# Attention loads on two queues in a ring of six, stores per two tiles, weight splits moved to the experts

## The reference, cut to what matters

```python
def _attn_ref(r, k, v, w, u):            # (4, 8, 768, 48): batch, head, position, width
    for t in range(S):
        cur = einsum('bhd,bhe->bhde', u[None] * kt, vt)
        y[:, :, t] = einsum('bhd,bhde->bhe', rt, state + cur)
        state = w[None, :, :, None] * state + einsum('bhd,bhe->bhde', kt, vt)

def _moe_ref(x, w_skip, w_gate, w1, w2): # x (3072, 384), 8 experts, hidden 1024
    keep = x @ w_skip > 0; e = argmax(x @ w_gate)
    y = softmax(x @ w_gate)[e] * (maximum(x @ w1[e], 0) @ w2[e])
    return x + y where keep, x elsewhere

def _moe2_ref(x, w1, w2, w3, w_out):     # 384 -> 1024 -> 1024 -> 384
    return (((x @ w1) * (x @ w2)) @ w3) @ w_out
```

## Time and profile before

| quantity | value |
|---|---|
| median of three runs | 710.27 us |
| the profiled execution, whole | 708.51 us |
| its span, first to last instruction | 706.4 us |
| TensorE busy | 640.1 us (91%) |
| VectorE, ScalarE, GpSimd busy | 291.5, 224.4, 157.4 us |
| packets under 512 B, of all | 79875 of 106784 |
| mean granted TensorE clock | 0.954 |

### The profile page before, as it was taken

One profiled execution on the slowest core, in us unless ns is written; L12 is line 12 of the kernel. 1 busy time (PEld: TensorE's weight loads), 2 busy tenths in 40 slices (PEclk: granted clock), 3 DMA queues, 4 the chain that ended last, 5 costly groups with the idle time before them and its releaser, 6 DMA issues. The chain is left out here.

```text
span 706.4 us, 15335 instructions
## 1 busy us (share of the span) xinstructions
PE 640.1 (91%) x6244; PEld 571.7 (81%) x6244; DVE 291.5 (41%) x458; ACT 224.4 (32%) x400; POOL 157.4 (22%) x188
## 2 busy tenths in 40 slices
PE   7568687697899989899988899999999999999997
PEld 6457587686666989899987788888888889888886
DVE  5335465463291765566652212322322323213222
ACT  2224243342233544455541411321322213213221
POOL 7425464570254233222221400000000000000000
PEclk9877897897999999999999999999999999999999
DMA  6666667673460663566530300200200200100001
GB/s 123 126 146 124 154 127 158 157 170 117 132 248 17 199 207 124 206 209 211 201 123 19 134 1 1 89 1 1 90 1 1 89 1 1 45 1 16 31 0 45
DMA packets 106784, 67.87 MB, mean 96 GB/s; under 512 B 79875, under 2 KB 101541, under 8 KB 106737
## 3 DMA queue, kind: packets, MB, share of 16 engines
q1 hardware_dynamic: 104688, 62.62, 31.9%
q0 software_dynamic: 2048, 4.58, 1.9%
HBM read 56.31 MB, written 12.58 MB: 98 GB/s over the span
## 5 line engine op out<-in xcount | busy, mean ns | idle before, releaser
L1273 PE MATMUL gl_pab<-gl_xT_hi,wm_lo 128*128 128x512 f32 x288 | 112.9, 392 | 0.0
L1273 PE MATMUL gl_pab<-gl_xT_lo,wm_hi 128*128 128x512 f32 x288 | 112.8, 392 | 0.0
L1273 PE MATMUL gl_pab<-gl_xT_hi,wm_hi 128*128 128x512 f32 x288 | 112.1, 389 | 0.0
L1353 DVE TENSOR_TENSOR gl_g_sb<-gl_a_sb,gl_pab 128x512 f32<-128x512 f32 x48 | 33.0, 688 | 186.8 <-ACT gl_a_sb L1330 186.8
L1330 ACT ACTIVATE gl_a_sb<-gl_pab 128x512 f32<-128x512 f32 x48 | 28.7, 599 | 185.1 <-PE gl_pab L1273 185.1
L1288 PE MATMUL gl_po<-gl_wf_hi,gl_g_hi 128*128 128x384 f32 x192 | 65.6, 342 | 0.7 <-DVE gl_g_lo L1355 0.7
L1288 PE MATMUL gl_po<-gl_wf_hi,gl_g_lo 128*128 128x384 f32 x192 | 64.7, 337 | 0.0
L1288 PE MATMUL gl_po<-gl_wf_lo,gl_g_hi 128*128 128x384 f32 x192 | 64.5, 336 | 0.0
L1273 PEld LDWEIGHTS gl_pab<-gl_xT_hi,wm_lo 128*128 128x128 f32 x288 | 54.0, 188 | 11.4
L1273 PEld LDWEIGHTS gl_pab<-gl_xT_lo,wm_hi 128*128 128x128 f32 x288 | 54.0, 188 | 10.5
L1273 PEld LDWEIGHTS gl_pab<-gl_xT_hi,wm_hi 128*128 128x128 f32 x288 | 54.1, 188 | 10.3
(11 more groups left out here) (192 smaller groups left out, 1246.5 us busy)
## 6 DMA issues: line engine op xcount, KB each, us to landing
ew_w_in<-in_moe_w SPq DMA_DIRECT2D x16, 1536.0 KB, 6.8
k_in<-in_k SPq DMA_DIRECT2D x48, 96.0 KB, 2.9
r_in<-in_r SPq DMA_DIRECT2D x48, 96.0 KB, 3.0
v_in<-in_v SPq DMA_DIRECT2D x48, 96.0 KB, 2.9
xbuf<-x_nat SPq DMA_DIRECT2D x48, 96.0 KB, 2.3
gl_x_in<-xbuf SPq DMA_DIRECT2D x12, 384.0 KB, 4.0
out<-gl_o_sb SPq DMA_DIRECT2D x12, 384.0 KB, 2.6
w_in<-in_moe_w SPq DMA_DIRECT2D x8, 512.0 KB, 4.0
```

Source lines behind the costliest of these rows:

```text
L1273: m = pe.matmul(p_ab[f % 2][w][:, :], a[:, w * KD + k, cols], b[t.slot][:, k, :], start=(k == 0 and n == 0), stop=(k == KD - 1 and n == 2))
L1353: dve.tensor_tensor(g_sb[f % 2][:, :], a_sb[f % 2][:, :], p_ab[f % 2][1][:, :], ALU.mult).then_inc(s_g, 1)
```

## The change

1. The hardware loop in attention is gone: all 24 tiles are written out, with constant addresses and constant counts. TensorE's `ready()` (a semaphore increment that nothing waits for) goes too.
2. k, r and v have rings of six tiles (`NB = 6`). SyncE loads k and r of tile m+5. The v loads are issued by ScalarE: eight DMAs ahead of its first instruction, then two per step for tile m+5, behind `kT_out`.
3. `x_nat` holds two tiles per pair of batches; the store moves both, once per two tiles.
4. `v_in` loses its padding between heads and `k_rev` shares the memory of `A_m`.
5. The `wm` weights are loaded and split in the experts: with experts 0 to 5 one block of 128x1024 each, into the buffers `w3_in` of the fold. SyncE issues the load behind that of w2, ScalarE does `wm_hi` behind `x_hi`, GpSimd does `wm_lo` behind the gather.

```diff
-        def schedule(eng, parts, lead, lag, extra=None):
-            for n in range(-lead, NS):
-                step(n // NS, n % NS)
-            with eng.Fori(1, NCH - 1) as c:
-                for j in range(NS):
-                    step(c, j)
-            for n in range(NS * (NCH - 1), NT + lag):
-                step(n // NS, n % NS)
+        def schedule(parts, lead, lag, extra=None):
+            for m in range(-lead, NT + lag):
                 for f, shift in parts:
+                    if 0 <= m + shift < NT:
+                        f(Tile(m + shift))
...
             def load_rk(t):
-                wait(sp, s_Tr, t.num(1, 1 - NS))
+                wait(sp, s_Tr, t.n + 1 - NB)
...
-            def load_v(t):
-                wait(sp, s_Y, t.num(1, 1 - NS))
-                wait(sp, s_vb, t.num(1, 1 - NS))
...
-            def store(t):
-                wait(sp, s_x, t.num(1, 1))
+            def store(t):
+                if t.a == 0:
+                    return
+                sp.wait_ge(s_x, t.n + 1)
                 for jj in range(2):
-                    sp.dma_start(xbuf[bass.ds(t.chunk(P, C * t.a + (2 * t.pr + jj) * S), C), :], x_nat[t.pr][half(jj), :]).then_inc(s_store[t.pr], 16)
+                    sp.dma_start(xbuf[b * S + P * t.c:b * S + P * (t.c + 1), :].rearrange("(a s) w -> s a w", a=2), x_nat[t.pr][half(jj), :, :]).then_inc(s_store[t.pr], 16)
-            schedule(sp, ((load_rk, 4), (load_v, 3), (store, -2)), 4, 2, extra)
+            schedule(((load_rk, 5), (store, -2)), 5, 2, extra)
...
         def _(act):
+            def load_v(t):
+                wait(act, s_Y, t.n + 1 - NB)
+                wait(act, s_vb, t.n + 1 - NB)
+                for jj in range(2):
+                    act.dma_start(t.v(half(jj), 0, W).rearrange("p (h d) -> p h d", d=D), rows_of(v, t, jj)).then_inc(s_vin[t.buf], 16)
+            for n in range(4):
+                load_v(Tile(n))
...
-            schedule(act, ((kT_out, 1), (new_state, -1), (xT_out, -1), (y_out, 0)), 1, 2, extra)
+            schedule(((kT_out, 1), (load_v, 5), (new_state, -1), (xT_out, -1), (y_out, 0)), 1, 2, extra)
...
             def x_out(t):
-                wait(dve, s_store[t.pr], t.chunk(64, 32 * t.a))
+                wait(dve, s_store[t.pr], 32 * t.c)
...
+        def wm_block(t):                              # in experts()
+            return isinstance(t.c, int) and t.num() >= 2 * KD
+                def load_wm(t):
+                    if wm_block(t):
+                        return
+                    wait(sp, fold.s_T, fold.KF)
+                    wait(sp, s_wmlo, t.num(1, -1))
+                    sp.dma_start(fold.w3_in[t.slot][:, :], wm[t.slot][bass.ds(t.turn(P), P), :]).then_inc(s_wmin[t.slot], 16)
-                rounds(sp, whole(sp, (load_w1, 1), (load_w2, 1)), 2, E, 0, 0)
+                rounds(sp, whole(sp, (load_w1, 1), (load_w2, 1), (load_wm, 0)), 2, E, 0, 0)
...
+                    pool.tensor_tensor(wm_part(wm_lo, t), fold.w3_in[t.slot][:, :].unsqueeze(1), wm_part(wm_hi, t), ALU.subtract).then_inc(s_wmlo, 1)
-                rounds(pool, whole(pool, (scatter, 0), (gather, 2)), 2, E, 1, 0)
+                rounds(pool, whole(pool, (scatter, 0), (gather, 2), (wm_lo_, 0)), 2, E, 1, 0)
...
+                    act.activation(wm_part(wm_hi, t), fold.w3_in[t.slot][:, :].unsqueeze(1), ACT.Copy).then_inc(s_wmhi, 1)
-                rounds(act, whole(act, (hidden_hi, 0), (w1_hi_, 1), (x_hi, 1)), 2, E, 1, 0)
+                rounds(act, whole(act, (hidden_hi, 0), (w1_hi_, 1), (x_hi, 1), (wm_hi_, 0)), 2, E, 1, 0)
...
+                pe.wait_ge(env["s_wmlo"], 2 * KD)     # ahead of the gated layers
```

More of the change, by code:

```diff
@@ L146, in attention @@
         v_bonus = [sb(f"v_bonus{i}", [P, H, D]) for i in range(2)]
-        x_nat = [sb(f"x_nat{i}", [P, W]) for i in range(2)]
+        x_nat = [sb(f"x_nat{i}", [P, 2, W]) for i in range(2)]
         xT = [sb(f"xT{i}", [P, KC, P]) for i in range(2)]
@@ L176, in attention, with __init__ @@
         s_acc, s_ssum, s_scaled = sem("s_acc"), sem("s_ssum"), sem("s_scaled")
[L177 removed]
         class Tile:
[L181 to L183 removed]
+            def __init__(self, n):
+                self.n, self.c, self.slot = n, n // NS, n % NS
                 self.a, self.pr = self.slot // 2, self.slot % 2
[L185 to L203, removed]
@@ L205, in schedule, with v, x @@
-        def schedule(eng, parts, lead, lag, extra=None):
-            def step(c, j):
+                self.frame = 2 * self.c + self.pr
+                self.makes_state, self.no_past = n < NT - 2, n < 2
+                self.buf, self.use = n % NB, n // NB + 1
+                self.r, self.k = r_in[:, self.buf, :, :], k_in[self.buf][:, :, :]
+            def v(self, rows, h, cols):
+                return v_in[self.buf][rows, h * D:h * D + cols]
+            def x(self, rows):
+                return x_nat[self.pr][rows, self.a, :]
@@ L250, in load_rk, with extra @@
                                  allow_slow_non_contiguous=True).then_inc(s_gates, 16)
[L252 to L254 removed]
+            def store(t):
+                if t.a == 0:
+                    return
+                sp.wait_ge(s_x, t.n + 1)
                 for jj in range(2):
[L256 to L268 removed]
+                    b = 2 * t.pr + jj
+                    sp.dma_start(xbuf[b * S + P * t.c:b * S + P * (t.c + 1), :].rearrange("(a s) w -> s a w", a=2), x_nat[t.pr][half(jj), :, :]).then_inc(s_store[t.pr], 16)
+            def extra(m, f):
+                if f is store and m == NT - NS:
                     fold.load(sp, [0])
@@ L329, in updates @@
             def updates(t):
-                if not t.makes_state():
+                if not t.makes_state:
                     return
[L332 to L335, removed]
-                    wait(pe, s_acc, t.chunk(2, 1))
-                else:
-                    wait(pe, s_ssum, t.chunk(2, 1))
-                ready()
+                v_loaded(pe, t)
+                if t.n:
+                    prev = Tile(t.n - 1)
+                    pe.wait_ge(s_ssum if prev.a else s_acc, prev.frame + 1)
                 for m in range(HP):
@@ L347, in own_rows @@
             def own_rows(t):
-                wait(pe, s_vin[t.slot], t.chunk(32, 32))
-                wait(pe, s_mask, t.num(1, 1))
-                ready()
+                v_loaded(pe, t)
+                wait(pe, s_mask, t.n + 1)
                 for s in range(2):
@@ L937, in experts @@
     NO = env["over_expert"].shape[1]
-    ident = env["ident"]
+    ident, fold = env["ident"], env["fold"]
+    wm, wm_hi, wm_lo = env["wm"], env["wm_hi"], env["wm_lo"]
     with ExitStack() as ctx:
@@ L961, in experts, with wm_part @@
         s_Y, s_new = sem("Y"), sem("new")
+        s_wmin, s_wmhi, s_wmlo = [sem(f"wmin{i}") for i in range(2)], sem("wmhi"), env["s_wmlo"]
+        def wm_block(t):
+            return isinstance(t.c, int) and t.num() >= 2 * KD
+        def wm_part(x, t):
+            return x[:, bass.ds(t.c + t.slot * KD, 1), :]
         class Over(Item):
```

220 lines of the change are left out of this document (107 added, 113 removed).

## The result

The changed kernel takes 688.62 us (median of 4 runs, 687.61 to 690.82), against 710.08 us for the kernel before in the same job (4 runs, 707.66 to 710.45): a ratio of 0.971, interval 0.968 to 0.974. It is 21 us faster, where 51 had been forecast, and lies above the range of 645 to 681 us.

A forecast was written before the change was run, and what follows sets the result against it. Attention was taken to be bound by SyncE's issuing queue, with TensorE next. From 708.5 us, attention gave -57.9 and the experts +7, so 657.6; the median's 1.8 more made 659, range 645 to 681 us.

The forecast's parts named there:

- Written out, and without `ready()`: Attention without the loop: 4.50 us a step (4.27 to 4.85), the low end if a 0.17 us weight-load wait goes.
- rival D: TensorE's instructions arrive late in attention, a 4.45 us stall plus low clock once in four steps: 45 us, 704; chance 0.05.
- 21 x 4.50: Attention's 21 steps after steps 0 and 1, at 4.50 us each: 94.5 us.
- SyncE's queue: Attention: fewer issues make 3.2 us a step, below TensorE's 4.44, so the queue no longer sets the pace.
- the stores: Attention: the 39.4 us that `x_out` waited for stores go, and with them the low clock.
- The DMA engines: Attention: the engines need 4.0 to 4.3 us a step, narrowly under TensorE's 4.44; no cost taken.
- rival B: The DMA engines become attention's bound, 4.9 us a step, 668 us, or 680 with late data; chance 0.16.
- ScalarE: Attention: v issues at 0.645 us each bring its step to 4.14 us, under 4.44; 0.05 us a step charged.
- rival E: Attention: an issue holds ScalarE until its data land, +65 us, 782 us; chance 0.02 with other ways to be slower.
- The start: Attention's start: eight v loads ahead of ScalarE's first work cost 0 to 5.2 us; +1.5 taken.
- The experts: `wm` loads make more gathers late, 4.5 us a case, splits cost nothing: +7 us, half of 13.5.

The follow-up runs named there:

- experiment 2: The changed kernel but with the hardware loop, `ready()`, the buffer layout and the ring of four kept: 673.78 us, ratio 0.950.
- experiment 11: The kernel of experiment 2 with TensorE's attention steps alone written out, the other four engines left in the loop: 687.09 us, ratio 0.970.
- experiment 9: The kernel of experiment 2 with two loop turns of eight tiles in place of four turns of four: 701.12 us, ratio 0.990.
- experiment 4: The changed kernel without the six 512 KB loads of `wm`; the splits stay and work on what is in the buffer: 686.54 us, ratio 0.968.
- experiment 1: The kernel before with attention written out and nothing else changed: 696.5 us, ratio 0.985.
- experiment 5: The kernel before with v loads on ScalarE and paired stores; loop kept, `wm` still split in attention: a gain of 4.2%.
- experiment 6: The kernel before with only the v loads moved to ScalarE, loop kept: a gain of 3.5%.
- experiment 7: The kernel before with only the stores paired, one per two tiles, loop kept: a gain of 1.8%.
- experiment 12: The kernel of experiment 5 with the two `wm` loads a turn issued by GpSimd in place of SyncE: 682.78 us, ratio 0.961.
- experiment 3: The changed kernel with r and v loaded only for the first six tiles: 677.2 us, ratio 0.954.
- experiment 8: The kernel before with only the `wm` loads and splits moved to the experts, loop kept: just above the expected 704 to 709 us.
- experiment 10: The changed kernel with a ring of four tiles in place of six: 685.75 us, ratio 0.968.

## Why the prediction was wrong

The step that failed is "*Written out, and without `ready()`*", which was given a low end (4.27 us a step) and no high one, and with it rival D, priced at 45 us and a chance of 0.05. Writing out is what costs: experiments 2 and 11 differ in nothing but TensorE's loop, and lie 13.3 us apart. D's mechanism came, more often and in smaller pieces than its six stalls of 4.45 us: eleven of up to 3.3 us and the low clock behind them, 28 us in place of 45.

Not all of these 28 are the change's doing. With the loop kept (experiment 2) the same 21 steps took 132.33 - 22.45 = 109.9 us, 15.4 more than the forecast's 94.5, nearly all of it at the stage's two ends. So about half of the miss is the writing out of the middle, and half that *21 x 4.50* charged every step as an undisturbed one, although the ends are written out in both kernels and the earlier trace rows is a stall at such an end.

The prediction had the evidence in the earlier trace rows, and weighed against it the rule of the Trainium skill, "Runtime: NRT & Kernel Launch", section "Instruction fetch mechanics", that fetch runs ahead in sequence and a taken branch breaks it. Measured, the branch back costs about 0.2 us where the body fits (experiment 2: steps of 4.68 and 4.65 us across the branch, 4.44 to 4.47 elsewhere from the second turn on), and in sequence the stream of 298 instructions in 4.44 us still came late eleven times. What the rule says of the branch came out where the body does not fit: 5.52 us in experiment 9.

The other terms, one by one:

- *SyncE's queue* and *the stores*: right. The 39.4 us of waits went, and undisturbed steps take 4.43 us against 4.44.
- *The DMA engines* (rival B): it falls. In experiment 2 they ran at 0.85 through 71 us, twelve steps in a row took 4.44 to 4.68 us, and nobody waited for them. That they never showed more than 88% was a misreading: the kernel before has 0.96 from 8 to 12 us.
- *ScalarE*: right. Its issue costs what SyncE's does, 1.30 / 2 = 0.65 us (first row below), and rival E falls with it.
- *21 x 4.50 = 94.5 us*: measured 122.9, by the stalls and the clock; 109.9 with the loop kept.
- *The start*, +1.5: +4.3 measured. Experiment 2, with four v loads ahead in place of eight, begins step 2 at 22.45, +2.4.
- *The experts*, +7: +6.2 measured. That the number fits is in part luck: it was half of a range from nothing to 13.5, and the mechanism was half right. TensorE's wait for the gather grew from 7.3 to 11.9 us, by the same number of cases, three, and not by more of them (second row below). The splits were costed at nothing; without the loads, in experiment 4, the experts still took 170.2 us, so they may be a part of it. Over all runs, the experts take 158.1 to 168.9 us where `wm` is split in attention (before and experiments 1, 5, 6, 7, 12), and 170.2 to 175.4 where beside them (after and 2, 3, 4, 8 to 11).

The two rows of the changed kernel, from ScalarE's queue behind kT_out, and from the waits of the experts:

```profile
108.75 1.30 ACTq L385 DMA_DIRECT2D v_in<-in_v  x2
```

```profile
PE ex_px L1037 <- DMA ew_x_in<-xbuf,ew_token: 11.9, 3, 4.7
```

Open: what decides that one piece of the stream is late and the next is not (the mean DMA share does not), and whether the stalls at the loop's entry and exit can be avoided, which wasn't tried, nor was the exit without the loads of w3 and w_out beside it.

## What to carry to other kernels

A written-out stage was not free here for an engine with many small instructions: count its instructions, and look in the profile for idle time that ends at "issue" in the middle of a group, and for packets of the instruction queue. If a loop's body is short enough that such packets cease, keep the loop. Here, taking stores out from behind loads and v off SyncE's queue gave most of the gain. Before moving a load and its splits to another stage, or a load to another queue, ask which in-order engine will stand behind its consumer there.

## What the runs showed of the hardware

VectorE's subtractions stand while GpSimd's run, in the splits beside the experts. These rows are the sums from 202 to 376 us of the changed kernel; before, VectorE's two groups were busy for 30.7 and 26.8 us:

```profile
L1131 DVE TENSOR_TENSOR ew_w_lo<-ew_w_in,ew_w_hi 128x768 fp32r<-128x768 f32 x32 | 37.9, 1184 | 7.6 <-ACT ew_w_hi L1098 6.8
...
L871 DVE TENSOR_TENSOR ew_w_lo<-ew_w_in,ew_w_hi 128x768 fp32r<-128x768 f32 x30 | 33.5, 1173 | 6.1 <-PEq L626 5.9
...
L1016 POOL TENSOR_TENSOR wm_lo<-w_in,wm_hi 128x1024 f32 (+1 forms) x6 | 14.4, 2398 | 0.2
```

VectorE's grew by 13.9 us, GpSimd's `wm_lo` sums to 14.4. The median of VectorE's instructions did not move (946 to 959 ns in both kernels); single ones rose to 3.4 us. There are six of these long ones, and each overlaps one of GpSimd's six subtractions; one pair of them in the timeline:

```profile
251.71 3.36 DVE L1131 TENSOR_TENSOR ew_w_lo<-ew_w_in,ew_w_hi 128x768 fp32r<-128x768 f32 x1
...
251.84 2.40 POOL L1016 TENSOR_TENSOR wm_lo<-w_in,wm_hi 128x1024 fp32r<-128x1024 f32 x1
```

The excess over 0.96 us is 2.40 us, GpSimd's whole duration. So while GpSimd subtracts, VectorE's subtraction stands.
